# A recurrence and two MLPs on one core: units of 64 tokens of all batches, one joined recurrence segment per chunk behind four MLP steps

## The reference

```python
# r, k, v, w, a, b: (batch 4, heads 8, tokens S = 768, D = 40)
for t in range(S):
    y[t] = r[t] @ state                                  # per batch and head, state is D x D
    Sa = state @ a[t]
    state = state * w[t] - outer(Sa, b[t]) + outer(v[t], k[t])
x = y as (3072 tokens, 320)
g = leaky_relu(x @ w_in)          # w_in 320 x 2048, slope 0.01
x = g @ w_out1                    # 2048 x 320
out = (sigmoid(x @ w_gate) * (x @ w_val)) @ w_out2       # 320 x 1536 twice, 1536 x 320
```

## Time and profile before

| | |
|---|---|
| median of 3 runs | 1132.85 us (1128.9 to 1137.99) |
| span of the profiled execution, first to last instruction | 1129.2 us |
| time of the profiled execution beside its span | none is given; the span is within 0.3 us of the fastest run |
| instructions | 36605 |
| busy: TensorE products / weight loads | 1072.3 us (95%) / 917.0 us (81%) |
| busy: VectorE / ScalarE / GpSimd | 595.8 us (53%) / 397.3 us (35%) / 146.4 us (13%) |
| chain that ended last | PE 89%, issue 4%, DVE 3%, ACT 1%, POOL 1% |

### The profile page before, as it was taken

How to read it: one execution, slowest core, us unless ns; L and a number is a source line. 1 busy time by engine, 2 the same in 40 slices (tenths; PEclk the granted TensorE clock), 3 DMA queues, 4 the chain that set the end, 5 groups by cost and what they waited for, 6 DMA issues and landing times.

```text
span 1129.2 us, 36605 instructions
## 1 busy us (share of the span) xinstructions
PE 1072.3 (95%) x16106; PEld 917.0 (81%) x16106; DVE 595.8 (53%) x1306; ACT 397.3 (35%) x782; POOL 146.4 (13%) x179
## 2 busy tenths in 40 slices
PE   2888979999999999999999999999999999999998
PEld 2777868888888887788788788888888888888887
DVE  7797786767676776667574224443223232323222
ACT  2142243344444443533343335542222222222222
POOL 6313030403122121303010000000000000000000
PEclk9977679999999999999999999999999999999999
DMA  5836363344335342434333024220201002020000
GB/s 176 252 103 151 68 129 80 82 110 123 85 75 134 89 108 62 125 90 100 64 110 79 9 91 145 80 89 1 61 1 57 5 1 61 1 61 1 24 1 23
DMA packets 133856, 87.62 MB, mean 78 GB/s; under 512 B 98274, under 2 KB 113634, under 8 KB 133700
## 3 DMA queue, kind: packets, MB, share of 16 engines
q1 hardware_dynamic: 126740, 62.85, 22.8%
q0 software_dynamic: 6960, 22.45, 6.6%
HBM read 66.39 MB, written 18.87 MB: 76 GB/s over the span
## 4 chain that ended last, share of the span: by engine, by line
PE 89%; issue 4%; DVE 3%; ACT 1%; POOL 1%; DMA 0%; SPq 0%; ACTq 0%; POOLq 0%; DVEq 0%
PE bank L808 16%; PE bank L858 12%; PE pair L858 12%; PE bank L823 4%; PE bank L878 4%; PE bank L876 4%; PE bank L877 4%; PE bank L824 4%; PE bank L825 4%; PE bank L894 3%; PE bank L783 2%; PE bank L760 2%; PE bank L774 2%; PE bank L630 2%; PE bank L828 2%
## 5 line engine op out<-in xcount | busy, mean ns | idle before, releaser
L1301 DVE TENSOR_TENSOR g_lo<-g_full,g_hi 128x512 fp32r<-128x512 f32 x168 | 125.3, 746 | 229.8 <-ACT g_hi L1064 229.6
L1064 ACT CAST g_hi<-g_full 128x512 fp32r<-128x512 f32 x168 | 104.3, 621 | 134.7 <-DVE g_full L1354 131.6
L808 PE MATMUL bank<-x_hi,w_up 128*128 128x512 f32 x480 | 134.7, 410 | 3.6 <-issue 3.6
L1057 ACT ACTIVATE g_full<-bank 128x512 f32<-128x512 f32 x96 | 57.5, 599 | 210.0 <-PE bank L808 204.7
L1256 DVE TENSOR_TENSOR t_unit<-t_unit,prod 128x126 f32<-128x126 f32 (+22 forms) x372 | 106.5, 286 | 12.8
L1252 DVE TENSOR_TENSOR prod<-t_unit,p_unit 128x126 f32<-128x126 f32 (+22 forms) x372 | 102.1, 275 | 20.1 <-DMA p_unit<-p_dram 7.0
L808 PEld LDWEIGHTS bank<-x_hi,w_up 128*128 128x128 f32 x480 | 85.4, 189 | 23.0 <-issue 4.5
L1354 DVE TENSOR_TENSOR g_full<-pair,h_sb 128x512 f32<-128x512 f32 x36 | 24.9, 692 | 112.7 <-PE pair L858 112.0
L808 PE MATMUL bank<-x_lo,w_up 128*128 128x512 f32 x288 | 82.1, 393 | 0.0
L823 PE MATMUL bank<-g_hi,w_dn 128*128 128x512 f32 x192 | 76.4, 398 | 0.4 <-DVE g_lo L1301 0.2
L824 PE MATMUL bank<-g_hi,w_dn 128*128 128x512 f32 x192 | 75.0, 391 | 0.0
(11 more groups left out here) (146 smaller groups left out, 2401.0 us busy)
## 6 DMA issues: line engine op xcount, KB each, us to landing
p_unit<-p_dram SPq DMA_DIRECT2D x48, 128.0 KB, 2.9
stage<-in_w_out POOLq DMA_DIRECT2D x7, 640.0 KB, 5.8
v_tok<-in_vT SPq DMA_DIRECT2D x12, 320.0 KB, 3.1
v_nu<-in_vN SPq DMA_DIRECT2D x24, 160.0 KB, 5.9
x<-y_sb SPq DMA_DIRECT2D x48, 80.0 KB
k_sb<-in_kF POOLq DMA_DIRECT2D x22, 160.0 KB, 3.4
v_sb<-in_vF SPq DMA_DIRECT2D x22, 160.0 KB
r_sb<-in_rF SPq DMA_DIRECT2D x22, 160.0 KB
```

Source lines behind the costliest of these rows:

```text
L808: last = nc.tensor.matmul(up_bank(m)[:], lhs, rhs, start=(e == 0), stop=(e == len(products) - 1))
L1064: nc.scalar.copy(g_hi[:, m % 2], g_full[:]).then_inc(g_hi_ready, 1)
L1301: nc.vector.tensor_tensor(g_lo[:, m % 2], g_full[:], g_hi[:, m % 2].bitcast(F32), ALU.subtract).then_inc(g_lo_ready, 1)
```

## The change

- A unit is now 64 tokens of all four batches. Its two chunks, n = 2t and 2t + 1, are the two halves of the batches at the same time; a chunk needs the state of chunk n - 2. The host lays the inputs out accordingly. The first two chunks have no state and the last two leave none, so their `sn`, state parts and `st` are left out.
- A window is one chunk: four MLP steps and then one joined segment of all recurrence groups: `rhs` begun, `sn` and `vrur` of the chunk before, `rhs` ended, `st` of the chunk before, `first`, `cross`, the scores (`a` four chunks ahead, `ka` one ahead, the state part of `y`), `y` ended for the chunk before, `ut`/`u`, `kb` of the next chunk. The first MLP step stands in window 6, so segments 0 to 5 stand ahead of it.
- In odd sequences the halves of the partitions are exchanged for r, v, `kb`, `sn`, `ut` and `u` (`side`), so that neighbouring products use other quarters of the array.
- `y` and `st` share bank 0 with the up products. `ut`/`u` and `sn` lie in the bank pair 4, 5. `vrur` and `u_feat` have a tile of their own (`vru`) beside `x_f`.
- The weights are loaded into the place where they stay, as float32, and split there; `stage` is gone. Pieces 0 and 1 are split in window 4, the others in windows 6 to 8.
- k and b are fetched per chunk; r and v are held once instead of twice.
- `fill` is gone. VectorE's columns, ScalarE's copies and SyncE's queue stand in new orders.

The core of the diff (where an order was rewritten, only the new one stands here; the old one is in the functions above):

```diff
-LAG = 18
+LAG = 24
...
+        raw_weights = ExitStack()
+        up_raw = [sb(raw_weights, f"up_raw{i}", [P, 5, GW]) for i in range(4)]
+        dn_raw = [sb(raw_weights, f"dn_raw{i}", [P, GT, DN]) for i in range(4)]
+        raw_weights.close()
         w_up = [sb(ctx, f"w_up{i}", [P, 5, GW], F32R) for i in range(4)]
         w_dn = [sb(ctx, f"w_dn{i}", [P, GT, DN], F32R) for i in range(4)]
         x_f = sb(ctx, "x_f", [P, 3 * BLK])
-        p_sb = sb(ctx, "p_sb", [P, 2, TQ, L])
-        first_units = ExitStack()
-        w_first = sb(first_units, "w_first", [P, 4, WN + 1])
-        first_units.close()
-        first_weights = ExitStack()
-        stage = sb(first_weights, "stage", [P, 4, 3 * GW])
-        first_weights.close()
+        vru = sb(ctx, "vru", [P, 3 * BLK])
...
-        BANKS = dict(rhs=((4, 5), (4, 5)), sn=((6,), (6,)), first=((7,), (7,)), a=((6,), (6,)), ka=((7,), (7,)),
-                     ut=((4,), (4,)), u=((5,), (5,)), st=((5,), (5,)), vrur=((6, 7), (6, 7)), y=((6,), (6,)),
-                     kb=((4, 7), (5, 6)))
-        TENSOR_ORDER = [("rhs", 0, 0), ("sn", 0, 0), ("first", 0, 0),
-                        ("a", 2, 0), ("ka", 1, 0), ("ut", 0, 0), ("u", 0, 0),
-                        ("st", 0, 0), ("vrur", 0, 0),
-                        ("rhs", 0, 1), ("y", 0, 0), ("first", 0, 1),
-                        ("a", 2, 1), ("ka", 1, 1), ("ut", 0, 1), ("u", 0, 1), ("sn", 0, 1),
-                        ("st", 0, 1), ("vrur", 0, 1),
-                        ("y", 0, 1),
-                        ("kb", 1, 0), ("kb", 1, 1)]
...
+        def mlp_step(n, s):
+            m = 4 * n + s - LAG
+            return m if 0 <= m < M1 else None
+        HAS = dict(rhs=NT, vrur=NT, st=NT - 2, first=NT, a=NT, ka=NT, y=NT, utu=NT, kb=NT)
+        BANKS = dict(rhs=(4, 5), vrur=(6, 7), st=(0,), first=(6,), a=(6,), ka=(7,), y=(0,), utu=(4, 5), kb=(6, 7))
+        SLOT_X = [("rhs", 0), ("vrur", -1), ("st", -1), ("first", 0)]
+        SLOT_Y = [("a", 4), ("ka", 1), ("y", -1), ("utu", 0), ("kb", 1)]
+        STEPS = range(-4, NT + 6)
+        def has(op, n):
+            return 0 <= n < HAS[op]
+        def has_state(n):
+            return 2 <= n < NT
+        turn_of, turns = {}, {i: 0 for i in SHARED}
+        turns_before_up, up_before = {}, {}
+        last_up = -1
+        for window in STEPS:
+            for s in range(4):
+                if mlp_step(window, s) is not None:
+                    last_up = mlp_step(window, s)
+                    turns_before_up[last_up] = turns[0]
+                for op, ahead in (SLOT_X + SLOT_Y if s == 3 else []):
+                    if has(op, window + ahead):
+                        for bk in BANKS[op]:
+                            turns[bk] += 1
+                            turn_of[op, window + ahead, bk] = turns[bk]
+                        up_before[op, window + ahead] = last_up
...
+            for which, bk in enumerate(BANKS[op]):
+                if bk != 5:
+                    wait(pe, bank_emptied[bk], turn(op, n, which) - 1)
+                if bk == 0:
+                    wait(pe, g_ready, up_before[op, n] + 1)
...
+            for n in range(-4, NT):
+                if n >= 0:
+                    fetch_k(pool, n + 2)
+                    fetch_b(pool, n + 4)
+                if chunk(n + 4):
+                    pool_a(pool, n + 4)
+                    pool_b(pool, n + 4)
+                if chunk(n + 2):
                     pool_k(pool, n + 2)
+                if n >= 0:
+                    fetch_a(pool, n + 5)
+                if n == -1:
+                    pool.wait_ge(p_low_loaded, 32)
+                    load_piece(pool, 0)
+                    load_piece(pool, 1)
+                elif n == 0:
+                    pool.wait_ge(t_loaded, 64)
+                    load_piece(pool, 2)
+                    load_piece(pool, 3)
+                elif n == 1:
+                    load_piece(pool, 4)
+                    load_piece(pool, 5)
+                elif n == 2:
                     load_piece(pool, 6)
                     load_piece(pool, 7)
...
+            for n in range(NT + 3):
+                if 2 <= n < NT + 2:
+                    store_y(sp, n - 2)
+                    load_v(sp, n - 1)
+                    load_r(sp, n - 1)
+                if n % 4 == 1 and n >= 5:
+                    load_x(sp, (n - 5) // 4)
+                if n >= 1:
+                    store_p(sp, n + 3)
+                if n % 2 == 0 and n >= 2:
+                    load_p_top(sp, (n + 2) // 2)
+                    load_p_low(sp, (n + 2) // 2)
+                load_w(sp, n + 5)
+                if n % 2 == 0 and n >= 2:
+                    load_v_nu(sp, n // 2)
+                if n % 2 == 1:
+                    load_v_tok(sp, (n + 1) // 2)
+                    store_t(sp, (n + 1) // 2)
+                    load_t(sp, (n + 1) // 2)
+                if n % 4 == 2 and n >= 10:
+                    store_o(sp, (n - 10) // 4)
...
+        def side(i, q):
+            return i if q % 2 == 0 else 1 - i
+        def state_to_y(n, q):
+            for i in range(2):
+                j = side(i, q)
+                last = nc.tensor.matmul(bank[bank_of("y")][half(i, D), q * L:(q + 1) * L], sn_sb[half(j, D), q],
+                                        r_sb[half(j, D), q], start=(q == 0), stop=False, skip_group_check=True)
+            return last
...
+        def pe_sn(pe, n):
+            if not chunk(n + 1):
+                emptied(pe, "utu", n)
+            pe.wait_ge(state_ready, n - 1)
             for q in range(TQ):
                 for i in range(2):
-                    last = nc.tensor.matmul(o[upper(i), q * D:(q + 1) * D], t_sb[upper(i), c, q, 0:C],
+                    last = nc.tensor.matmul(pair[half(side(i, q), D), q % 2, DM // 2 + q // 2 * D:DM // 2 + (q // 2 + 1) * D],
+                                            st_sb[half(i, D), n % 2, q], ident[half(i, D), half(i, D)],
+                                            start=(not chunk(n + 1)), stop=True, skip_group_check=True)
+                if q >= TQ - 2:
+                    last.then_inc(sn_multiplied[q % 2], 1)
...
-        FILL = {("kb", -1): 2, ("sn", 0): 56,
-                ("first", 0): 2, ("cross", 0): 2, ("ut", 0): 4, ("vrur", 0): 6,
-                ("first", 1): 2, ("cross", 1): 2, ("ut", 1): 2, ("st", 1): 2, ("vrur", 1): 10, ("kb", 0): 4,
-                ("first", 2): 2, ("cross", 2): 4, ("ut", 2): 4, ("vrur", 2): 4,
-                ("first", 3): 2, ("cross", 3): 2, ("ut", 3): 2, ("st", 3): 1, ("vrur", 3): 6, ("kb", 1): 6,
-                ("first", 4): 2, ("cross", 4): 4}
-        def fill(pe, place, n):
-            for _ in range(FILL.get((place, n), 0)):
-                nc.tensor.matmul(bank[0][:, 0:P], ident[:], ident[:], start=True, stop=True)
...
+            for n in STEPS:
+                for s in range(4):
+                    m = mlp_step(n, s)
                     if m is not None:
                         up_products(pe, m)
+                        if m > 0:
+                            down_products(pe, m - 1)
+                    if s == 3:
+                        if chunk(n):
+                            pe_rhs_begin(pe, n)
+                        if has_state(n - 1):
+                            pe_sn(pe, n - 1)
+                        if chunk(n - 1):
+                            pe_vrur(pe, n - 1)
+                        if chunk(n):
+                            pe_rhs_end(pe, n)
+                        if has("st", n - 1):
+                            pe_st(pe, n - 1)
+                        if chunk(n):
+                            pe_first(pe, n)
+                        if chunk(n):
                             pe_cross(pe, n)
+                        pe_scores(pe, n + 4, n + 1, n - 1)
+                        if chunk(n - 1):
+                            pe_y_end(pe, n - 1)
+                        if chunk(n):
                             pe_ut_u(pe, n)
+                        if chunk(n + 1):
+                            pe_kb(pe, n + 1)
...
+                place, raw = w_up[grp], up_raw[grp]
+                if i > 0:
+                    act.wait_ge(x_lo_ready, 3)
+                    act.wait_ge(w_split, i - 1)
+                nc.scalar.copy(place[:, 0:2], raw[:, 3:5])
+                nc.scalar.copy(place[0:K2, 2], raw[0:K2, 2])
+                nc.scalar.copy(x_part(0)[K2:P].bitcast(F32R), raw[K2:P, 2]).then_inc(w_hi_ready, 1)
             else:
-                nc.scalar.copy(w_dn[grp][:, :, 0:DM],
-                               stage[:, i % 4, 0:GT * DM].rearrange("p (f d) -> p f d", d=DM)).then_inc(w_hi_ready, 1)
+                place, raw = w_dn[grp], dn_raw[grp]
+                nc.scalar.copy(place[:, :, 2 * P:DM], raw[:, :, DM:DM + K2])
+                nc.scalar.copy(place[:, :, 0:2 * P], raw[:, :, DM + K2:DN]).then_inc(w_hi_ready, 1)
...
+            for first in range(4):
+                dve_decay(dve, first)
```

(45 more changed lines are left out.)

840 lines of the change are left out of this document (341 added, 499 removed).

## The result

The changed kernel takes 1255.36 us (median of 4 runs, 1251.78 to 1264.37) where the kernel before, on the same chip, takes 1132.28: 1.1124 times as long, interval 1.1053 to 1.1194. The span of the profiled execution is 1253.6 us. The forecast of 1136 us, and its range up to 1162, were far too low.

The account below looks back on a forecast made before the run. TensorE was taken to bound the middle and end, round trips and VectorE the start. Start 180 + MLP steps 348.2 + recurrence beside them 204 + rest 399.8 = 1132.0 us of span, 1136 as median; range 1110 to 1162.

Parts of the forecast that it names:

- In the middle the engine is busy throughout and the clock whole: Middle windows, MLP steps beside recurrence: TensorE would stay busy and keep its full clock, so no half-clock cost was added.
- The middle: MLP steps with recurrence beside them: windows of 25.7 us, recurrence 204 us where 222.8 was.
- g_lo: Down products in each middle window: TensorE waits for VectorE's late g_lo, taken as 1.0 us, bounds 0 and 2.5.
- The start: Segments 0 to 5, before the first MLP step: 180 us, between ends 171 (full clock) and 191 (half clock).
- Exchanged halves: Small products in the segment: sn and y's state part use all array quarters in turn; sn 0.52 us for 0.8.
- rival (3): Segment products: exchanged halves don't overlap, sn and y keep their price; +0.6 us a chunk, 1148 us; chance 0.08.
- Gap: Between first and cross in each segment: ScalarE's copy is uncovered, 0.64 us with both handovers.
- rival (2): Down products: columns ahead of g_lo run later, TensorE waits every window; decides over 1.5 us a chunk; about 1160; chance 0.28.
- Pure steps and second MLP: Behind the last segment: 24 pure MLP steps of 3.63 us, then the second MLP in 396 us as before.
- No cost for `fill`: Start: fill is gone and the half clock will be common there, within the 180 us taken.
- r and v singly buffered at no cost: Loads of r and v: needed 16 us after issue; without MLP steps VectorE's columns cover them; no cost.
- The weights' pieces and their loads: Windows 6 to 8: six weight pieces split there, one pair in an odd window without slack, +3.5 us; loads in place free.

Follow-up runs that it names:

- e2: The changed kernel with its joined segment cut in two, the first half behind the second MLP step of a window: 1158.81 us, 1.030 times the kernel before.
- e6: The changed kernel with VectorE's masks and state operations moved ahead of the third- and fourth-quarter columns, only where no MLP steps run: 1220.78 us, 1.085 times the kernel before.
- e4: The kernel before the change with its fill products removed: 1127.21 us, 1.002 times the kernel before.
- e11: The changed kernel with its joined segment cut in four parts behind the MLP steps of a window: 1190.04 us, 1.053 times the kernel before.
- e8: e2 with SyncE's queue reordered and VectorE forming g_lo ahead of scans and columns in every quarter: 1187.77 us, 1.054 times the kernel before.
- e13: e2 with the middle's loads of r, v, w and both token forms of v cut to one or two partitions: 1166.89 us, 1.035 times the kernel before.

## Why the prediction was wrong

**The step that failed** is the sentence "In the middle the engine is busy throughout and the clock whole". The middle missed by 95.5 us. Of that 43.2 is the half clock (the busy time of the joined segments less that of the halves), 31.2 unnamed waits that the sum didn't have, nearly all for packets of instructions, 5.0 is g_lo (23.0 against 18 x 1.0), 4.6 small waits, and 11.5 is what the products take even at e2's clock over the 526.4 of the sum (555.9 less 18 x 1.64 for the gap and g_lo). I gave no price to a run of 10 us of small products, though the one from 326.31 to 329.96 in the trace before, between two steps, is 3.65 us. The busy share of the earlier trace rows, 493.8 of 505.7 us, came with few stalls; the sum itself put 1.64 us of them into each new window and still took the clock as whole.

**The start** was mis-sized, 206.1 for 180, beyond its end of 191. The first masks came at 79.3 us for 72.5. From masks to y it took 8.9 to 9.5 us where I had 6.2 and, as the other end, 10.1. From y to the masks: 16.5 to 22.5 us in odd windows for 14.3, and 19.2 and 21.0 for 16.6 in even ones. The rows above show why: columns of 1.14 and 1.17 us in place of 0.29 (a mean as in the earlier trace rows) beside GpSimd's operations, and p_unit there 13.9 us after the end of y, where the sum had 11.2. The order itself, columns ahead of masks, was in my sum, and I took it as given; e6 shows that another order takes 28.9 us off. By the Trainium skill, SBUF - State Buffer, "SBUF: two separate sides", a VectorE operation with two SBUF inputs and a GpSimd operation that reads SBUF shut each other out for a whole instruction; the rows agree: GpSimd's scaling of b runs from 123.03 to 124.21 and of k from 124.17 to 125.39, and the two columns beside them last that long.

**The rest, by its steps.** Exchanged halves: right as far as sn shows it. The full-clock segment's 9.91 us busy has sn in 0.44 us, under the 0.52 of the sum, and rival (3) didn't happen. Gap: right, 0.62 us, 11.0 in all. g_lo: near, 23.0 us for 18; rival (2) had the mechanism, but a mean wait of 23.0 / 18 = 1.3 us is under its point of decision, and its 1160 would still have been 95 us short. Pure steps and second MLP: right, 396.1. No cost for `fill`: the prediction had the half clock common in the start without it, and e4's start has less clock but is 3.8 us shorter. "r and v singly buffered at no cost": wrong in the start, 16.9 us of waits for r there. The weights' pieces and their loads don't appear among TensorE's waits in the middle.

## What to carry to other kernels

Before many small groups are joined to save edges between them, ask what the large products between them did for the small ones: here the steps of 512-column products between them kept TensorE at 2.4 GHz and gave the next instructions time to arrive, and taking them away cost 43 + 24 us in a middle where the forecast saving was 19. Price a stall by the products behind it too: e11's 23.4 us of waits for r went with 21.6 us of busy time. Cutting the joined segment in two gives the clock back; dense products put inside it cost what they return. In a stretch without cover (the start), follow one chunk through each engine's written order: a mask that 20 columns are written ahead of costs their time in each window.

## What the runs showed of the hardware

The granted clock stayed at 0.50 for 6 us in which TensorE's busy share was 1.00 (the 1-us windows above), and came back 1.5 us ahead of the next 512-column product. The Trainium skill, TensorE: Matmul & The Clock Gate, "What's actually happening", says that the clock follows how busy the engine has been; the falls of the changed kernel agree, since each stands behind stalls that sum to 1 us or more, and those 6 us at a busy share of 1.00 don't. The same products cut into runs of 5 us had 0.99 in e2 and in one run of 10 us 0.91, but e8's runs of 5 us, with 63.5 us of idle time in the middle, had 0.95.

TensorE also stands still, up to 2.5 us at a time, where its next 256 records are late: 29 of 30 unnamed waits of the changed kernel's middle end 1.2 to 1.5 us behind a packet of the instruction queue, 26.8 us of such waits are left in a middle of halves against 7.2 before, and they are as long with light data traffic as with heavy (e13).
